# Padding that moves every TensorE tile to a multiple of 512 bytes, one wait of ScalarE taken out, and w_out split one step later

## What is computed

```python
for t in range(S):                                   # attention, 4 batches x 8 heads x 768 steps, 48 wide
    state = alpha[:, :, t, :, None] * state + k_t outer v_t
    y[:, :, t] = q_t @ state
x = y as (3072, 384)
h = x @ w_in;  g = relu(h) ** 2;       x = g @ w_out      # first layers, 384 -> 2048 -> 384
h = x @ w2_in; g = h * sigmoid(h);     out = g @ w2_out   # second layers, the same shapes
```

## Time and profile before

| what | value |
|---|---|
| median of 3 runs | 894.65 us |
| profiled execution, own time | 893.18 us |
| span of its instructions | 891.6 us |
| TensorE matmul busy | 875.2 us, 98% of the span |
| VectorE busy | 540.8 us, 61% |
| ScalarE busy | 437.7 us, 49% |
| chain that ended last | 93% on TensorE |

### The profile page before, as it was taken

The page is one execution under the profiler, slowest core; times in us unless marked ns, Lnnn a source line. Parts: engine busy times, 40 slices in busy tenths (PEclk is TensorE's granted clock), DMA queues, the critical chain, the costliest instruction groups (busy, mean ns, idle before and its releaser), DMA issues.

```text
span 891.6 us, 17615 instructions
## 1 busy us (share of the span) xinstructions
PE 875.2 (98%) x6834; PEld 712.2 (80%) x6834; DVE 540.8 (61%) x1072; ACT 437.7 (49%) x770; POOL 104.1 (12%) x127
## 2 busy tenths in 40 slices
PE   7999989999999999999999899999999999999998
PEld 6777768788878887888888688888888888888898
DVE  7688876677767667663435546545754445766620
ACT  4765644455446444544566644445433436544510
POOL 2454300000000000000453003003030003000000
PEclk9999999999999999999999999999999999999999
DMA  9995334233333332300413360000130000110010
GB/s 155 223 241 129 90 70 122 66 81 101 70 82 86 104 71 65 102 19 26 153 36 73 62 159 10 0 1 1 43 100 0 1 1 1 35 36 1 1 47 28
DMA packets 134203, 60.03 MB, mean 67 GB/s; under 512 B 81824, under 2 KB 129312, under 8 KB 134112
## 3 DMA queue, kind: packets, MB, share of 16 engines
q1 hardware_dynamic: 130800, 58.14, 28.1%
q10 hardware_dynamic: 3312, 0.69, 0.6%
HBM read 45.02 MB, written 9.44 MB: 61 GB/s over the span
## 4 chain that ended last, share of the span: by engine, by line
PE 93%; DVE 3%; issue 1%; ACT 1%; DMA 1%; ACTq 0%; DVEq 0%
PE z_ps L1144 21%; PE h_ps L1173 21%; PE h_ps L1130 20%; PE z_ps L1209 11%; PE jobs L1209 7%; PE jobs L1229 3%; PE jobs L1005 1%; PE jobs L1038 1%; PE jobs L1107 1%; PE jobs L1016 1%; PE jobs L1115 1%; PE h_ps L1229 1%; DMA nat_k<-in_k 1%; DVE decay L1700 1%; PE jobs L994 1%
## 5 line engine op out<-in xcount | busy, mean ns | idle before, releaser
L1427 ACT ACTIVATE g<-h_ps 128x512 f32<-128x512 f32 x96 | 57.4, 598 | 178.9 <-PE h_ps L1130 176.8
L1521 ACT ACTIVATE sum<-sum 128x512 f32<-128x512 f32 x96 | 60.6, 631 | 140.7 <-DVE sum L1868 117.3
L1868 DVE TENSOR_TENSOR sum<-h_ps,sum 128x512 f32<-128x512 f32 x120 | 82.8, 691 | 61.1 <-PE h_ps L1173 58.2
L1807 DVE TENSOR_TENSOR g_lo<-g,g_hi 128x512 fp32r<-128x512 f32 x96 | 67.5, 704 | 85.4 <-ACT g L1433 85.4
L1130 PE MATMUL h_ps<-x_hi,win_hi 128*128 128x512 f32 x288 | 115.1, 399 | 1.3 <-ACT g L1427 0.8
L1144 PE MATMUL z_ps<-g_hi,wout_hi 128*128 128x512 f32 x282 | 115.1, 408 | 0.0
L1130 PE MATMUL h_ps<-x_hi,win_lo 128*128 128x512 f32 x288 | 112.3, 390 | 0.0
L1130 PE MATMUL h_ps<-x_lo,win_hi 128*128 128x512 f32 x288 | 112.1, 389 | 0.0
L1144 PE MATMUL z_ps<-g_hi,wout_lo 128*128 128x512 f32 x282 | 110.6, 392 | 0.0
L1144 PE MATMUL z_ps<-g_lo,wout_hi 128*128 128x512 f32 x282 | 110.6, 392 | 0.0
L1173 PE MATMUL h_ps<-s_hi,t_hi 128*128 128x512 f32 x264 | 104.5, 396 | 3.2 <-DVE sum L1868 1.8
(11 more groups left out here) (169 smaller groups left out, 1553.1 us busy)
## 6 DMA issues: line engine op xcount, KB each, us to landing
z_scratch<-z_sb SPq DMA_DIRECT2D x18, 256.0 KB, 2.8
pre<-z_scratch SPq DMA_DIRECT2D x18, 256.0 KB, 3.9
v_sb<-in_v SPq DMA_DIRECT2D x44, 96.0 KB, 2.7
out_x<-z_stage SPq DMA_DIRECT2D x80, 48.0 KB, 1.7
nat_a<-in_alpha SPq DMA_DIRECT2D x40, 88.0 KB, 2.3
nat_k<-in_k SPq DMA_DIRECT2D x40, 88.0 KB, 2.5
nat_q<-in_q SPq DMA_DIRECT2D x40, 88.0 KB, 2.3
nat_a<-in_alpha SPq DMA_DIRECT2D x40, 80.0 KB, 2.2
```

The source lines that it names most:

```text
L1427: nc.scalar.activation(g[f % 2][:], h_ps[f % 2][:], ACT.Relu).then_inc(act_made, 1)
L1521: nc.scalar.activation(at[:], at[:], ACT.Silu).then_inc(silu_made, 1)
L1807: nc.vector.tensor_tensor(low, g[f % 2][:], high.bitcast(F32), ALU.subtract).then_inc(g_lo_made, 1)
L1868: nc.vector.tensor_tensor(to[:], h_ps[(PRODUCTS * n + r) % 2][:], other[:], ALU.add).then_inc(summed, 1)
```

## The change

Two unused tensors are added (96 bytes and 384 bytes per partition) and a third grows from 128 to 512 bytes. With them the tensors from `nat_a0` to `decay0`, and all of those from `w_ring` on, begin at 0 modulo 512 instead of 416 and 32; so do `s_hi`, `s_lo`, `t_hi0` and `t_lo0`. `ident`, `all_held` and `ones` stay where they are. Slices inside the attention tiles begin at multiples of 192 or 256 bytes from their tensor's start, as before.

The first ring tile (slot 0) no longer waits for `z_step`; slots 1 to 3 wait for 94, 95 and 96 as before. `v_group` gives group 0 chunk 1 instead of 1, 2 and 3, and group n = 1 to 7 chunks 2n and 2n + 1 instead of 2n + 2 and 2n + 3 (none in group 7).

```diff
 def v_group(n):
 
-    return {0: (1, 2, 3)}.get(n, (2 * n + 2, 2 * n + 3) if n < GROUPS - 1 else ())
+    return (2 * n, 2 * n + 1) if n else (1,)
...
         redo = sb("redo", [1, 1], mybir.dt.int32)
+        sb("gap2", [P, 24], F32)
...
             decay = [sb(f"decay{i}", [ROWS, SCANS], F32, one) for i in range(2)]
+            sb("gap3", [P, 96], F32, one)
             w_ring = sb("w_ring", [P, RING * DM], F32, one)
...
-        sb("gap0", [P, 32], F32)
+        sb("gap0", [P, 128], F32)
...
                 elif slot < 4:
                     act.wait_ge(g_lo_made, STEPS)
-                    act.wait_ge(z_step, STEPS - (0, 2, 1, 0)[slot])
+                    if slot:
+                        act.wait_ge(z_step, STEPS - 3 + slot)
```

## The result

| | before | after |
|---|---|---|
| median | 894.56 us (894.02 to 895.22, 4 runs) | 881.91 us (879.24 to 882.49, 4 runs) |
| ratio, 95% interval | | 0.9852 (0.9836 to 0.9867) |
| profiled execution | 893.18 us | 879.24 us |
| span of its instructions | 891.6 us | 877.6 us |

The change takes 12.65 us off the median, where 10.3 were forecast. Lines of the new kernel are two higher than those of before on TensorE and GpSimd (L1173 is now L1175) and three higher on VectorE (L1868 is now L1871); on ScalarE they are two higher up to the edit of the wait and three behind it (L1533 is now L1536).

A forecast was written before the change was run, and what follows sets the result against it. TensorE, with matmuls in flight for 875.2 of 891.6 us, was the bound. Padding 6.6 plus waits 3.7 made 10.3 us off 893.18, so 882.9; with 1.47 up to the median, 884.4 us; range 881 to 893.5.

The forecast's parts named there:

- The padding, second layers: TensorE, second layers: common start offsets bring 1,520 matmuls from 231.04 to 226.7 ns, 6.6 us; bounds 0 and 3.8.
- the natural experiment: Same 69 matmuls: group 8, tiles at 416 like `s_hi`, 228.7 ns each; group 9, pair 1 at 32, 231.2.
- The last stage: 192 matmuls of 384 columns at 173.3 ns, both operands taken to be at 32 already: gain 0.
- Rival 1: Second layers: padding does little or nothing, alternation itself makes distances irregular; 891.0 us, up to 892.5; chance 0.16.
- Rivals 2 and 3: Every matmul: starts at 0 remove 13.3 ns, 839 us, chance 0.10; or cost 4.5 ns, 897 us, chance 0.07.
- The waits: Group 0: slot 0's wait removed and fewer `low_v` before P3's sum, 3.7 us together; 2.2 if the clock falls.
- first wait: Group 0, TensorE waiting for ScalarE's second spread before P7: shrinks from 1.54 to about 0.05 us.
- second: Group 0, TensorE waiting for VectorE's sum of P3 before P4: 1.2 us left in place of 1.94.
- The moved chunks: Groups 1 to 7: cost nothing; group 7's two extra fit, VectorE's sum of P3 about 0.4 us later but covered.
- lost without cover: Group 7: 0.4 us, were C12 not ready two microseconds ahead of P4.
- The loads: DMA queue: its list is not touched; no gain or loss was forecast for loads.
- its own case: The forecast of 884.4 us, chance 0.62: 882 with the first layers' 1.9, 887.5 with group 8's rate or lower clock.

The follow-up runs named there:

- e1_align_only: The kernel before with the padding alone, old waits and old `v_group`: 888.29 us, ratio 0.9919.
- e7_weights_384: The changed kernel with everything streamed at 0 and nearly all large feed-forward weights at 384 modulo 512: 899.51 us in one run.
- e4_all_at_32: The changed kernel with all the same tiles at 32 modulo 512 in place of 0: 882.13 us, ratio 0.9848.
- e10_best: The changed kernel with no chunk moved into group 7, and group 0's second spread put before `copy_z`, its `low_v` after C12's sum: 881.19 us.
- e9_v_only: The kernel before with `v_group` alone changed, slot 0's wait and addresses as before: 892.73 us in one run.
- e2_waits_only: The kernel before with slot 0's wait and `v_group` changed, all addresses as before: 889.92 us, ratio 0.9936.

## Why the prediction was right, and where it was not

**The padding, second layers (6.6 us forecast): right.** The cause was the mismatch, the level reached was the 226.7 ns of the earlier trace rows, and the natural experiment in the earlier trace rows had pointed to it. Measured: 5.8 us from group 1 on; the rest of 6.5 us is lost in two places, groups 7 and 8 (0.38 us) and around 746 and 769 us (0.36). The last stage gave 0.1 us. The prediction had both its operands at 32; by the order in which `sb` reserves space `keep_hi2`, `keep_hi3` and `keep_lo1` to `keep_lo3` lay at 416, so a small part of its matmuls did have a mismatch. The Trainium skill, page "SBUF — State Buffer", section "Operand start alignment", calls its rule one "about legality, not speed" and adds that its runs timed nothing, so it doesn't speak against an effect, as the prediction had it; its section "Who interferes with whom" says that "PE and ACT never wait on anyone", and by this the padding would have been worth nothing to TensorE. That sentence doesn't cover what the offsets of TensorE's own two operands do here: 226.8 ns a matmul in `e1_align_only`, 231.7 in `e7_weights_384`.

**Rival 1 (the alternation alone makes the distances irregular) fell** with `e4_all_at_32` (the same alternation of products and pieces, regular) and `e7_weights_384` (irregular in the first layers without a change of offset). It stays true of the stretch behind a small job only: there equal offsets don't help.

**Rivals 2 and 3 (a start at 0 takes away 13.3 ns, or costs 4.5) fell**: at 0 and at 32 a matmul takes the same 226.7 to 226.8 ns. The 13.3 ns beyond the columns stay.

**The waits (3.7 us forecast): right, term by term.** The second spread starts 0.53 us after the last first-layer matmul has ended (0.6 forecast); first wait 0.09 us (0.05); second 0.99 (1.2); clock kept. Group 0 is 4.01 us shorter in the profiles, some 0.14 of that from the padding (3.87 with the waits alone). In medians the edits gave 5.4 us; what the 1.5 us more are is open; the clock, as told above, may be a part.

**The moved chunks (forecast at nothing): a small miss.** The step said "VectorE needs 2 x 0.5 us and has 0.77 us idle there". I took 0.5 us from group 0, where GpSimd does nothing, and said that GpSimd's list isn't touched. Its list isn't, but its work lies in that very stretch, 4.57 us of it in the timeline above, and the two `low_v` took 3.09 us instead of 1.0. What it cost is 0.38 us in groups 7 and 8 together, and `e10_best`, with no chunk in group 7, has it back. That this is near the "0.4 us" that I named as lost without cover is chance: that sum had VectorE late by 0.4 us, not by two microseconds, and no irregular stretch. The Trainium skill's page "SBUF — State Buffer" says in "Who interferes with whom" that a VectorE instruction with two SBUF inputs contends with GpSimd's reads, and here the trace agrees, 0.55 against 1.55 us. At before's addresses less of it shows: groups 7 and 8 take 15.96 and 15.77 us in `e9_v_only`, as before, and 15.96 and 15.91 us in `e2_waits_only`.

**The loads (no term in the sum): the step that was missing.** The prediction said of the DMA queue only that its list is not touched, and gave the stage before the first layers nothing. But the padding moves the attention tiles too, and I looked at them only as TensorE's operands. They are also where q, k, alpha and v are loaded to, in pieces of 192 bytes. DMA view of the first 10 us, before:

```profile
DMA packets 7274, 1.36 MB, mean 136 GB/s; under 512 B 7274, under 2 KB 7274, under 8 KB 7274
...
nat_a<-in_alpha SPq DMA_DIRECT2D x4, 96.0 KB, 5.0
...
v_sb<-in_v SPq DMA_DIRECT2D x2, 96.0 KB, 6.4
```

and after:

```profile
DMA packets 9544, 1.78 MB, mean 178 GB/s; under 512 B 9544, under 2 KB 9544, under 8 KB 9544
...
nat_a<-in_alpha SPq DMA_DIRECT2D x4, 96.0 KB, 3.1
...
v_sb<-in_v SPq DMA_DIRECT2D x4, 96.0 KB, 3.3
```

The attention of the first unit runs alone up to the first feed-forward step and hangs on these loads. The last load on the chain that ends at 30 us (critical view of 0 to 30 us), before:

```profile
3.17 5.92 DMA nat_k<-in_k
```

and after:

```profile
0.93 2.86 DMA nat_a<-in_alpha
```

Before, the chain is held by loads until 9.1 us (to 18.4 us in `e9_v_only`), after, only until 3.8 us, as in all ten profiles with the tiles at 0 or 32. The jobs themselves didn't get faster: the 16 matmuls at L1086 (after: L1088) take 1.08 us in both. Behind this stage no loads show: from there to group 0 the two profiles differ by the stretch at the lower clock alone (1.48 against 1.56 us). That step begins at 30.17, 30.04, 28.91 and 29.09 us (mean 29.55) in the four profiles with the tiles at 416, and at 27.25 to 28.62 (mean 27.70) in the ten with them at 0 or 32: 1.85 us. Part of the spread inside each set goes with the moment at which the clock rises for good (7 to 15 us), and whether the faster loads bring that forward as well wasn't separated.

**The sum.** 10.3 us were forecast. What the profiles show is 6.0 us for the padding in the second layers and the last stage (with 0.14 in group 0), 3.9 for the waits and 1.85 for the start, 11.7 us in all; the median moved by 12.65. The last 0.9 us aren't traced to a step. The median of 881.91 lies inside the stated range, but 0.1 us below the 882 to 887.5 that the prediction gave its own case, and the start, which was missing there, is more than that.

## What to carry to other kernels

Look at start addresses modulo 256. In these matmuls what TensorE streams and its weights should begin at the same offset; 0, 32 and a difference of 256 did equally well. The loads of 192-byte pieces were slower into tiles at 416 than at 0 or 32, perhaps because the pieces lie across a boundary there. When tiles are moved, list everyone who touches them, the DMAs too, not only the engine for whose sake it is done. And price a moved VectorE instruction from a stretch in which GpSimd is as busy as at the new place.

## What the runs showed that was not expected

**The rate of small loads into SBUF changed with the address of their tiles.** Windows of 3 to 7 us, before, and after:

```profile
3.00:7.00 4.00, 2.20 (x9) 1.41 (x9) 1.94 (x6) 1.49 (x2) 1.44 (x3) 1.00 1.44 177
```

```profile
3.00:7.00 4.00, 3.07 (x14) 2.60 (x15) 2.46 (x7) 1.49 (x2) 1.44 (x3) 1.00 1.24 247
```

All four profiles with these tiles at 416 modulo 512 show 177 or 178 GB/s here, all ten with them at 0 or 32 show 239 to 247. At 416 every 192-byte piece of q, k and alpha crosses a multiple of 256 (it begins 160 bytes past one), at 0 and 32 none does. (The pieces of v lie 192 bytes apart, and some of them cross at each of these offsets.) The comparison of `e2_waits_only` with `e4_all_at_32`, which differ in gaps alone, is the cleanest. The Trainium skill's page "DMA: Bandwidth & Descriptors", in "How a descriptor splits into AXI transactions", says of reads that a transaction must start at a 256-byte boundary; if the same held for writes, such a piece would need two transactions and not one, which would fit. No run shows the transactions. No run varied the size of the pieces, so that the boundary is the cause, and not some other property of 416, is argued and not shown.

**A mismatch costs TensorE 4.4 to 5.7 ns a matmul, averaged over matched neighbours too**: means of 231.2 ns at a difference of 128 and 231.7 at 32, with the mismatch in the products alone, 232.4 at 384 where every matmul has it (groups 1 to 5 of `e7_weights_384`), 226.8 at 0 and 256. Why a difference of addresses between the two operands should matter at all, none of the runs tells.
